# Attention kernel, tile loop: both head groups' attention products in one run, with one copy and one subtraction

## The reference

```python
scores = scale * np.matmul(q, k.transpose(0, 1, 3, 2))      # 4 batches, 8 heads, 576 x 576, 64 per head
mask = (rel >= 0) & (rel < window)                          # window = 128
scores = np.where(mask, scores + bias[None], -1000000000.0)
attn = np.exp(scores - np.max(scores, axis=-1, keepdims=True))
attn = attn / (np.sum(attn, axis=-1, keepdims=True) + 1e-09)
x = np.matmul(attn, v)                                      # then heads side by side: 2304 x 512
...
h = x @ w_in                                                # 512 -> 1024
solu = h * sm                                               # sm: softmax of h
ln = (solu - mu) / np.sqrt(var + 1e-06) * g_ln
x2 = ln @ w_out                                             # 1024 -> 512
...
out = (silu(x2 @ w_gate) * (x2 @ w_val)) @ w_out            # 512 -> 1536 -> 512
```

## Time and profile before

| | us |
|---|---|
| median of 3 runs | 760.61 (759.18 to 761.05) |
| the profiled execution, own time | 762.61 |
| its span, first to last instruction | 760.8 |
| busy: TensorE, VectorE, ScalarE, GpSimd | 730.1, 487.7, 427.2, 394.6 |
| mean granted TensorE clock | 0.991 of full speed |

### The profile page before, as it was taken

One profiled execution on the slowest core, in us unless ns is written; L12 is line 12 of the kernel. 1 busy time (PEld: TensorE's weight loads), 2 busy tenths in 40 slices (PEclk: granted clock), 3 DMA queues, 4 the chain that ended last, 5 costly groups with the idle time before them and its releaser, 6 DMA issues.

```text
span 760.8 us, 13425 instructions
## 1 busy us (share of the span) xinstructions
PE 730.1 (96%) x4800; PEld 690.7 (91%) x4800; DVE 487.7 (64%) x873; ACT 427.2 (56%) x872; POOL 394.6 (52%) x408
## 2 busy tenths in 40 slices
PE   5888999999999999999999999999999999899998
PEld 5766888888888888889999999999999989799998
DVE  4677776777777777764685555555555599735451
ACT  6798766777777667556444434444343387245340
POOL 4586444444444445387656885967677926200000
PEclk9899999999999999999999999999999999899999
DMA  8644343433333331320522233433426664985832
GB/s 310 222 133 145 112 168 124 137 113 110 110 110 114 129 129 35 119 97 29 197 74 94 79 139 119 146 113 114 148 100 228 218 219 157 324 285 190 275 110 83
DMA packets 48285, 111.37 MB, mean 146 GB/s; under 512 B 3952, under 2 KB 29296, under 8 KB 48240
## 3 DMA queue, kind: packets, MB, share of 16 engines
q1 hardware_dynamic: 48240, 110.78, 42.3%
HBM read 76.55 MB, written 34.21 MB: 146 GB/s over the span
## 4 chain that ended last, share of the span: by engine, by line
PE 79%; DVE 9%; ACT 3%; POOL 3%; issue 3%; DMA 2%; SPq 0%; DVEq 0%; POOLq 0%; ACTq 0%
PE banks L561 33%; PE banks L709 14%; PE banks L547 11%; PE banks L523 11%; PE banks L509 3%; PE banks L494 2%; PE banks L485 2%; PE banks L486 2%; PE banks L533 1%; ACT fold L743 1%; DVE p_own L1036 1%; POOL st_sums L1396 1%; DVE p_prev L1037 1%; DVE lnt_lo L1082 1%; POOL fold L1298 1%
## 5 line engine op out<-in xcount | busy, mean ns | idle before, releaser
L561 PE MATMUL banks<-xs_hi,w_hi 128*128 128x384 f32 x504 | 169.0, 335 | 3.4 <-DVE v_sum L1135 1.5
L561 PE MATMUL banks<-xs_hi,w_lo 128*128 128x384 f32 x504 | 168.4, 334 | 0.0
L561 PE MATMUL banks<-xs_lo,w_hi 128*128 128x384 f32 x504 | 168.4, 334 | 0.0
L1288 POOL TENSOR_TENSOR k_lo<-qk_raw,kq 64x512 fp32r<-64x512 f32 x35 | 44.8, 1280 | 109.0 <-ACT kq L722 109.0
L561 PEld LDWEIGHTS banks<-xs_hi,w_hi 128*128 128x128 f32 x504 | 94.6, 188 | 5.2 <-DVE v_sum L1135 1.8
L561 PEld LDWEIGHTS banks<-xs_lo,w_hi 128*128 128x128 f32 x504 | 94.6, 188 | 0.0
L561 PEld LDWEIGHTS banks<-xs_hi,w_lo 128*128 128x128 f32 x504 | 94.6, 188 | 0.0
L709 PE MATMUL banks<-lot_hi,wo_hi 128*128 128x384 f32 x252 | 85.5, 339 | 3.5 <-DVE v_sum L1135 3.5
L547 PE MATMUL banks<-lnt_hi,wout_hi 128*128 (+1 forms) x288 | 86.9, 302 | 1.1 <-ACT x_out L722 0.6
L709 PE MATMUL banks<-lot_lo,wo_hi 128*128 128x384 f32 x252 | 85.2, 338 | 0.0
L709 PE MATMUL banks<-lot_hi,wo_lo 128*128 128x384 f32 x252 | 85.1, 338 | 0.0
(11 more groups left out here) (100 smaller groups left out, 1794.7 us busy)
## 6 DMA issues: line engine op xcount, KB each, us to landing
qk_raw<-in_qk SPq DMA_DIRECT2D x36, 768.0 KB, 4.3
lot_raw<-unit_scratch SPq DMA_DIRECT2D x63, 384.0 KB, 4.4
unit_scratch<-st_sums SPq DMA_DIRECT2D x18, 576.0 KB, 4.4
unit_scratch<-st_even SPq DMA_DIRECT2D x18, 384.0 KB, 2.5
unit_scratch<-st_odd SPq DMA_DIRECT2D x18, 384.0 KB, 3.2
w_raw<-in_wb SPq DMA_DIRECT2D x12, 512.0 KB, 4.3
v<-in_v SPq DMA_DIRECT2D x18, 256.0 KB, 2.7
x_scratch<-x_out SPq DMA_DIRECT2D x18, 256.0 KB, 2.2
```

The lines of the kernel that those rows point to most:

```text
L561: last = mm(ps[n % 2], w_of[l][:, k * P:(k + 1) * P], x_of[r][:, k * HALF:(k + 1) * HALF], start=start and k == 0 and i == 0, stop=k == 1 ...
L1288: nc.gpsimd.tensor_tensor(k_lo[k, g, :, odd, :], qk_raw[k, g, :, 2 * odd, :], kq[k, g, :, 3 * odd, :], ALU.subtract).then_inc(k_lo_done, 1)
```

## The change

`attend` now does both groups of a tile in one run of 32 records, into all 512 columns of the bank, at the place where group g = 1 stood: at the beginning of the step of its own tile. The copy and the subtraction handle 512 columns at once. The products, copy and subtraction of group g = 0 in the step before go away, so the layer product in front of them now has 18 records in one run (`range(0, 6)`), and behind it the layer-norm transposes of the second half and the probability transposes of g = 1 follow each other directly. The semaphores `x_ready`, `x_hi` and `x_done` count tiles instead of groups.

```diff
-        def x_views(part, g, odd):
+        def x_views(part, odd):
-            return xt[part][:, odd, 2 * g:2 * g + 2, :], ps_x[:, 0:256].rearrange("p (a n) -> p a n", a=2)
+            return xt[part][:, odd, :, :], ps_x.rearrange("p (c n) -> p c n", c=CM)
...
             def load_v(t, odd):
-                wait(sp, x_ready, 2 * t)
+                wait(sp, x_ready, t)
...
-            def attend(t, g, odd):
-                u = 2 * t + g
-                pe.wait_ge(masked, 2 * u + 1)
+            def attend(t, odd):
                 pe.wait_ge(v_in[odd], arrivals(t, odd))
-                wait(pe, x_done, u)
-                for pair in range(2):
+                wait(pe, x_done, t)
+                for c in range(CM):
+                    g, pair = c // 2, c % 2
                     for of_v, of_p in ((odd, p_own), (1 - odd, p_prev)):
-                        if of_p is p_prev and pair == 0:
-                            pe.wait_ge(masked, 2 * u + 2)
+                        if pair == 0:
+                            pe.wait_ge(masked, 4 * t + 2 * g + (1 if of_p is p_own else 2))
                         for half in range(2):
...
                 if cur:
-                    attend(t, 1, odd)
+                    attend(t, odd)
...
                 if prev:
                     transpose_ln(t - 1, 0, 1 - odd)
                 if x2:
-                    layer1_out(gx, f + 1, range(0, 4), spare)
+                    layer1_out(gx, f + 1, range(0, 6), spare)
                 if is_at(t, -1) or early:
                     keep_warm(WARM[6])
-                if att:
-                    attend(t + 1, 0, 1 - odd)
-                if is_at(t, -1) or early:
                     transpose_probs(t + 1, 1)
                 if prev:
                     transpose_ln(t - 1, 1, 1 - odd)
-                if x2:
-                    layer1_out(gx, f + 1, range(4, 6), spare)
                 if att and not is_at(t, -1) and not early:
                     transpose_probs(t + 1, 1)
...
                 if cur:
                     exp_hidden(t, odd)
-                if att:
-                    x_hi_part(t + 1, 0, 1 - odd)
...
-                wait(dve, x_ready, u - 1)
+                wait(dve, x_ready, t)
...
                 if early:
                     unfold(t + 1, 1)
-                    x_lo_part(t + 1, 0, 1 - odd)
                 if cur:
                     make_solu(t, odd)
                 if att and not early:
-                    x_lo_part(t + 1, 0, 1 - odd)
                     unfold(t + 1, 1)
```

More of the change, by code:

```diff
@@ L495, in transpose_probs @@
                 last.then_inc(pt_ready, 1)
-            def attend(t, g, odd):
-                u = 2 * t + g
-                pe.wait_ge(masked, 2 * u + 1)
+            def attend(t, odd):
                 pe.wait_ge(v_in[odd], arrivals(t, odd))
-                wait(pe, x_done, u)
-                for pair in range(2):
+                wait(pe, x_done, t)
+                for c in range(CM):
+                    g, pair = c // 2, c % 2
                     for of_v, of_p in ((odd, p_own), (1 - odd, p_prev)):
-                        if of_p is p_prev and pair == 0:
-                            pe.wait_ge(masked, 2 * u + 2)
+                        if pair == 0:
+                            pe.wait_ge(masked, 4 * t + 2 * g + (1 if of_p is p_own else 2))
                         for half in range(2):
-                            head = 4 * g + 2 * pair + half
-                            last = mm(ps_x[HD * half:HD * (half + 1), pair * P:(pair + 1) * P],
+                            head = 2 * c + half
+                            last = mm(ps_x[HD * half:HD * (half + 1), c * P:(c + 1) * P],
                                       v[:, of_v, head * HD:(head + 1) * HD], of_p[:, g, 2 * pair + half, :],
@@ L516, in hidden @@
                 if n == 0 and chunks[0] == 0:
-                    pe.wait_ge(x_done, 2 * t + 2)
+                    pe.wait_ge(x_done, t + 1)
                     wait(pe, solu_done, t)
@@ L586, in period @@
                     pe.wait_ge(masked, 4 * TILES)
-                    pe.wait_ge(x_done, 2 * TILES)
+                    pe.wait_ge(x_done, TILES)
                 if n < 9:
@@ L745, in exp_scores, with x_hi_part @@
                 last.then_inc(exp_done, 1)
-            def x_hi_part(t, g, odd):
-                act_e.wait_ge(x_ready, 2 * t + g + 1)
+            def x_hi_part(t, odd):
+                act_e.wait_ge(x_ready, t + 1)
                 wait(act_e, h_ready, 2 * t - 2)
-                copy(*x_views(0, g, odd)).then_inc(x_hi, 1)
+                copy(*x_views(0, odd)).then_inc(x_hi, 1)
             def exp_hidden(t, odd):
@@ L841, in step @@
                 if is_at(t, 0):
-                    x_hi_part(t, 1, odd)
+                    x_hi_part(t, odd)
                 if att:
@@ L883, in step @@
                 if is_at(t, TILES - 1):
-                    act_e.wait_ge(x_done, 2 * TILES)
+                    act_e.wait_ge(x_done, TILES)
                     xs_hi_part(0, X_ORDER[0][0])
@@ L928, in first_step @@
                 piece(2)
-                x_hi_part(0, 0, 0)
                 piece(3)
@@ L1038, in unfold, with x_lo_part @@
                                         ALU.mult).then_inc(masked, 1)
[L1040 to L1043, removed]
+            def x_lo_part(t, odd):
+                dve.wait_ge(x_hi, t + 1)
+                out, in_ = x_views(1, odd)
+                nc.vector.tensor_tensor(out, in_, x_views(0, odd)[0], ALU.subtract).then_inc(x_done, 1)
             def max_hidden(t, n, odd):
@@ L1158, in step @@
                 if cur and not is_at(t, 0):
-                    x_lo_part(t, 1, odd)
+                    x_lo_part(t, odd)
                 early = is_early(t)
@@ L1222, in first_step @@
                 unfold(0, 1)
-                x_lo_part(0, 0, 0)
                 piece(2)
                 piece(3)
-                x_lo_part(0, 1, 0)
+                x_lo_part(0, 0)
             run(dve, step, 2, first_step)
```

## The result

The changed kernel takes 772.99 us (median of four runs, 772.49 to 774.81) where the kernel before takes 759.89 (757.60 to 761.05) beside it: 1.018 times as long, with a 95% interval of 1.015 to 1.0211. It is 13.1 us slower; 12.7 were forecast.

A forecast was written before the change was run, and what follows sets the result against it. A chain over VectorE and GpSimd, from the first probability transposes to the second, balanced with TensorE's work beside it, was taken to bound the step. 760.6 + 0.2 + 11.3 + 0.5 + 0.7 = 773.3 us; range 770.0 to 777.0.

The forecast's parts named there:

- The short part: From first to second probability transposes of a step: stays 4.85 to 5.11 us, TensorE waiting some 1.4 us in it.
- The long part: From second probability transposes to the next first ones: grows from 12.70 to 13.58 us, 0.87 a step.
- the first steps: Before t=3: longer attention ahead of the hidden layer, partly won back later; +0.2 us (-1.0 to +1.4).
- The grouping rule: Copy and subtraction: larger operations help a saturated engine; by this alone the step would be 0.16 us shorter; priced at nothing.
- rival C: First steps: lower clock lasts through the moved products and work behind them; much slower, 776.3 us; chance 0.08.
- t=17: The moved group comes here too, but covers an earlier wait for `p_prev`: +0.5 us (0.3 to 0.9).
- the end of the loop: At t=18: six layer products now stand ahead of the transposes feeding `lnt_lo`; 0.7 us later (0 to 0.8).
- A: In the loop: TensorE's work sets the step and the short part falls to 3.5 us; 753 us; chance 0.05.
- B: In the loop: the chain shrinks by a few tenths, about 0.8 us come back each step; 762 us; chance 0.06.
- D: In the loop: the larger copy delays the exponentials, so the chain begins late; 0.3 us a step, 777.5 us; chance 0.07.

The follow-up runs named there:

- e6: Changed kernel with group g = 0's products back in the step before; single copy, single subtraction and joined transposes kept; 760.75 us, 1.0004.
- e11: Changed kernel with eight of the sixteen moved records (one chunk) back in the step before; 768.88 us, 1.011.
- e4: Changed kernel with VectorE's sums of the second group put right behind `unfold` of the first, ahead of the maximum and `lnt_lo`; 763.93 us, 1.004.
- e7: Changed kernel with the copy and the subtraction made in two halves of 256 columns; products still in one run; 773.24 us, 1.0162.
- e1: Changed kernel with two chunks of layer products put back between the layer-norm transposes and the second probability transposes; 773.99 us, 1.0183.
- e3: Changed kernel with the last two chunks of the layer product moved ahead of the second transposes; 766.28 us, 1.0073.
- e9: As e3, with the next tile's first-group scores also moved in front of the second probability transposes; 759.09 us, 0.9977.
- e12: As e9, but with one of the eight layer-product chunks put behind the second probability transposes; 760.11 us, 0.9989.
- e10: As e6, with one more layer-product chunk moved ahead of the second transposes, seven ahead and one behind; 757.81 us, 0.9969.
- e5: Kernel before the change, with the same move of VectorE's sums as in e4; 767.70 us, 1.0087.
- e13: Changed kernel with forty dummy TensorE products between the two transpose runs of the very first step (t = -1); 777.68 us, 1.0222.

## Why the prediction was right, point by point

*What bounds the kernel.* The decisive step was to see in the earlier trace rows that the second transposes start 0.14 us behind GpSimd, in a page that shows TensorE 96% busy. After confirms it with 4.99 us again, e6 and e11 by taking the edit back, e4 from the other side by shortening the chain.

*The short part.* Forecast 4.85 to 5.11 us; measured 4.83 to 5.10 in all fourteen steps. TensorE's work in it was put at 3.5, by distances of starts; the view says 3.81 to 3.85, because it also counts the modelled tail of the last product before each of the two waits (0.28 us for a layer product, 0.66 for the transposes, where the next start would follow after 0.12 and about 0.4). So the waits shown come to 1.0 to 1.3 instead of 1.4, though the work is about what was thought. The waiting was taken to be one, on `fold`; in fact 0.25 of it stands on `lnt_lo`, the input of the layer-norm transposes, which I had not placed in time. Neither changes the time, as the chain sets the end.

*The long part.* Forecast 0.87 a step, measured 12.70 to 13.57. Thirteen of them are 11.3; the second transposes of t=16 stand at 318.75 before and 331.22 after, and those 12.47 are the first steps' 1.20 and 11.3. The sixteen records are as dear here as there, and the copy and subtraction took 598 and 692 ns (forecast 588 and 685, from the earlier trace rows) and are hidden:

```profile
L716 ACT ACTIVATE xt_hi<-banks 128x512 fp32r<-128x512 f32 x18 | 10.8, 598 | 7.7 <-PE banks L508 7.6
L1034 DVE TENSOR_TENSOR xt_lo<-banks,xt_hi 128x512 fp32r<-128x512 f32 x18 | 12.4, 692 | 9.4 <-ACT xt_hi L716 9.4
```

*The grouping rule.* By its first half (larger operations help) the step should have been shorter; e7 and after show no gain in grouping (1.0162 and 1.018, each inside the other's interval, and the same steps). The condition that the Trainium skill (Perfetto Trace Analysis, Optimizing Scalar/DVE Operations) puts on it, a saturated engine, isn't met by either: VectorE is busy 63% of the span, ScalarE 56%.

*The term that was mis-sized: the first steps.* Forecast +0.2 (from -1.0 to +1.4); the first layer product, at t=3, starts at 74.27 before and 75.47 after: +1.2. The hidden layer of t=0 is 2.36 us late. My 1.36 for the longer attention was priced at the full clock; most of it ran at the lower one, which the earlier trace rows already showed for before's. The profile of e1, whose first steps are those of after, separates the two: there the clock was back at 1.00 by 24.5, before the attention. From the first attention product to the hidden layer it takes 3.39 us in e1, 4.65 in after and 2.28 in before, so some 1.1 us are the longer attention (a little more at the full clock, since before's began at the lower one) and nearly 1.3 the clock. That was rival C, and its mechanism was there in part; but later first steps win back about 1.2 of the 2.36. Where the lower clock begins and ends varies from one execution to the next: with the same order of work there, the hidden layer of t=0 starts between 28.09 and 29.44 in the profiles of after, e1, e3, e4, e9 and e12, and the first layer product between 74.95 and 75.47. So the term lies at +0.7 to +1.2 rather than at +0.2; how much of it is the clock and how much the order of work stays open, since e1 has its first layer product 0.9 late too, with another stretch at the lower clock (0.51 from 44.9 to 48.4) that after doesn't have. In taking the middle of two bounds I gave the gain of the later steps more weight than any row did.

*t=17 and the end of the loop.* Forecast +0.5 and +0.7; the layer product of t=17 is 0.36 later than the sum so far (+12.83 in all), that of t=19 another 0.54 less 0.26. The 0.26 are a gain that I hadn't forecast, between t=17 and the start of the second stage (337.7 before, 350.3 after, +12.6). The end of the loop waits for `lnt_lo` as forecast:

```profile
361.83 0.28 PE L546 MATMUL banks<-lnt_hi,wout_lo 128*128 128x256 f32 x1
362.81 0.38 PE L546 MATMUL banks<-lnt_hi,wout_hi 128*128 128x256 f32 x1 [0.70 <-DVE lnt_lo L1073]
```

At this point (349.70 in before) after is 13.11 us late, and at the start of the last stage too (620.5 and 633.6).

*The last stage.* The two profiled executions end only 10.4 us apart, since before's lost time in this stage to the clock:

```profile
633.60:771.20 137.60, 131.44 (x757) 130.80 (x755) 78.35 (x87) 60.42 (x86) 17.88 (x8) 1.00 0.59 210
```

```profile
620.50:760.80 140.30, 133.96 (x757) 133.32 (x755) 77.71 (x87) 60.35 (x86) 18.10 (x8) 0.98 0.60 206
...
660.00:680.00 20.00, 18.44 (x92) 18.44 (x93) 9.96 (x12) 8.41 (x14) 3.56 (x3) 0.83 0.98 355
```

The last stage took between 136.5 and 140.9 us in the profiles of all kernels here, and not in an order that any change explains. Two things in it go with its length: the clock, and one wait of TensorE for `v_sum`. With a clock of 1.00 and a wait of 1.5 us it took 136.5 (e9), with 1.00 and 2.4 us 137.6 (after), with 0.98 and 3.5 us 140.3 (before). That is why medians of whole executions and sums of steps agree only to about 2 us; the forecast had taken 2.0 off the profiled time for the median, and the medians differ by 13.1, as the loop does.

*The rivals.* A (faster, TensorE's work sets the step) is excluded by the unchanged short part and by e1. B (no difference) by the unchanged chain. C happened in part and in the first steps only; in the loop the clock stayed at 1.00 through waits of 0.9 and 0.25 us a step. D (a dearer step) by the long part at 13.57.

## What to carry to other kernels

An engine that is 96% busy may still be waiting for a chain on others which is just as long as the work beside it; cut the loop at the two ends of that chain and look whether the stretch shortens when TensorE has less to do in it. Work that stands between such a pair of points is cover and costs nothing there, and its whole duration when it is moved elsewhere: so move work into a stretch of that kind only up to its length (e10), and before moving any out ask what takes its place. The name on the wait is that of the last member only; moving independent work about (e1) changes the name and not the time.

## What the hardware showed that I had not expected

*A tiny VectorE operation lasts as long as GpSimd's.* `pden` on VectorE (128x4, in SBUF) takes 0.12 to 0.17 us when GpSimd is idle or about to end. Where GpSimd is inside `kq`, a `tensor_tensor`, it lasts until 0.03 us behind GpSimd's end. From t=3 on that is 0.57 us with 0.54 left (12 cases in before; 0.16 or 0.17 in the other 16), 0.33 with 0.30 to 0.31 left (13 cases in e4), and 0.54 to 0.66 with 0.51 to 0.63 left (25 cases in e5). The profile books it as busy time of VectorE, so it shows as no wait at all. The Trainium skill (SBUF — State Buffer, Who interferes with whom) says that VectorE and GpSimd share one pair of ports as an exclusive lock, that a `tensor_scalar` can take it, and that whichever issues first blocks the other wholly for its instruction; the trace agrees in all these cases. So an instruction of such a chain is best put where GpSimd is idle or nearly done. The same place in VectorE's order isn't the same moment for GpSimd: in t=10 `kq` starts 0.85 us behind the first transposes in e4 and 1.40 in e5, and the moved `pden` takes 0.33 and 0.66.

*A dummy product of 128 columns (f32) is two records.* Forty of them show as 80 records in e13, which start from 16.64 on, 0.112 us apart, and the next work starts at 25.57: 0.223 us a product, twice what one record suggests.

*The clock of the first steps moves about.* The same instructions in the same order gave starts of the hidden layer 1.35 us apart from one execution to the next (above). The first layer product of e6 and of e10, whose first steps are alike as well, stands at 75.32 and 73.73. Differences of that size at the beginning of a single profile are not evidence for an edit.
